# A tile of y kept in SBUF, and VectorE in GpSimd's place in the second layer: a float32 attention and two-layer kernel on one Trainium2 core

## What is computed

```python
scores = scale * np.matmul(q, k.transpose(0, 1, 3, 2))      # decayed causal attention, no softmax
attn = np.matmul(scores * Dmat, v)
x = attn.transpose(0, 2, 1, 3).reshape(2304, 512)
xn = x / rms(x) * rms_g                                     # first layer: 512 -> 1536 -> 512
g = xn @ w_gate
y = (g * sigmoid(g) * (xn @ w_val)) @ w_out
h = y @ w_in                                                # second layer: 512 -> 2048 -> 512
p = np.where(h >= 1, h, np.where(h <= -1, 0, (h + 1) ** 2 / 4))
out = p @ moe2_w_out
```

## Time and profile before

| | us |
|---|---|
| median of 3 runs | 904.11 |
| lowest and highest | 901.40, 905.42 |
| the profiled execution's own time | 900.61 |
| its span, from the first to the last instruction | 898.8 |
| TensorE matmul busy | 870.4 (97%) |
| VectorE, ScalarE, GpSimd busy | 571.9, 464.2, 251.9 |
| mean granted TensorE clock, share of full speed | 0.998 |

### The profile page before, as it was taken

One profiled execution on the slowest core, in us unless ns is written; L12 is line 12 of the kernel. 1 busy time (PEld: TensorE's weight loads), 2 busy tenths in 40 slices (PEclk: granted clock), 3 DMA queues, 4 the chain that ended last, 5 costly groups with the idle time before them and its releaser, 6 DMA issues.

```text
span 898.8 us, 17947 instructions
## 1 busy us (share of the span) xinstructions
PE 870.4 (97%) x7448; PEld 848.8 (94%) x7448; DVE 571.9 (64%) x799; ACT 464.2 (52%) x732; POOL 251.9 (28%) x172
## 2 busy tenths in 40 slices
PE   6898999999999999999999998999999999999998
PEld 5787999999999999999999988999999978999998
DVE  3599866477953653622242577766567879888884
ACT  2556654445654555511231457877778846433331
POOL 0236763446764664000040422404042000000000
PEclk9999999999999999999999999999999999999999
DMA  9984132333336336334633134233326673444442
GB/s 259 234 248 142 54 104 91 101 100 100 101 100 240 101 100 211 133 106 134 207 103 132 54 132 152 106 128 126 132 112 217 200 237 118 119 140 118 140 119 71
DMA packets 113329, 124.09 MB, mean 138 GB/s; under 512 B 6784, under 2 KB 85760, under 8 KB 113248
## 3 DMA queue, kind: packets, MB, share of 16 engines
q1 hardware_dynamic: 113248, 122.95, 43.5%
HBM read 80.45 MB, written 42.47 MB: 137 GB/s over the span
## 4 chain that ended last, share of the span: by engine, by line
PE 79%; DVE 7%; DMA 5%; ACT 3%; issue 2%; POOL 2%; SPq 1%; DVEq 0%; ACTq 0%
PE pair L727 14%; PE pair L729 14%; PE pair L728 14%; PE pair L825 6%; PE pair L827 6%; PE pair L826 6%; PE pair L888 5%; PE pair L890 5%; PE pair L889 5%; DMA a_kt<-ktok 4%; PE pair L858 1%; DVE cb L1496 1%; PE pair L859 1%; PE pair L860 1%; DVE wq L1528 1%
## 5 line engine op out<-in xcount | busy, mean ns | idle before, releaser
L727 PE MATMUL pair<-xc,wc 128*128 128x288 f32 x672 | 199.4, 297 | 0.6 <-ACT cp L1014 0.4
L728 PE MATMUL pair<-xc,wc 128*128 128x288 f32 x672 | 198.2, 295 | 0.0
L729 PE MATMUL pair<-xc,wc 128*128 128x288 f32 x672 | 197.6, 294 | 0.0
L1014 ACT ACTIVATE cp<-pair 128x576 f32<-128x576 f32 x160 | 103.4, 647 | 156.3 <-PE pair L729 150.2
L1679 POOL TENSOR_TENSOR wc<-wt,wc 128x512 fp32r<-128x512 f32 x84 | 122.6, 1483 | 92.2 <-ACT wc L947 86.6
L727 PE MATMUL pair<-xc,wr 128*128 128x288 f32 x448 | 133.6, 298 | 6.8 <-ACT cp L1014 6.3
L728 PE MATMUL pair<-xc,wr 128*128 128x288 f32 x448 | 132.2, 295 | 0.0
L729 PE MATMUL pair<-xc,wr 128*128 128x288 f32 x448 | 131.7, 294 | 0.0
L727 PEld LDWEIGHTS pair<-xc,wc 128*128 128x128 f32 x672 | 125.9, 187 | 1.6 <-issue 1.5
L729 PEld LDWEIGHTS pair<-xc,wc 128*128 128x128 f32 x672 | 126.6, 188 | 0.0
L728 PEld LDWEIGHTS pair<-xc,wc 128*128 128x128 f32 x672 | 126.2, 188 | 0.0
(11 more groups left out here) (124 smaller groups left out, 1702.6 us busy)
## 6 DMA issues: line engine op xcount, KB each, us to landing
b_scratch<-cb SPq DMA_DIRECT2D x32, 576.0 KB, 2.9
a_scratch<-cb SPq DMA_DIRECT2D x24, 576.0 KB, 2.9
av_r<-a_scratch SPq DMA_DIRECT2D x8, 1728.0 KB, 8.3
wt<-wB SPq DMA_DIRECT2D x72, 128.0 KB, 2.9
bt<-b_scratch SPq DMA_DIRECT2D x28, 256.0 KB, 2.8
bt<-b_scratch SPq DMA_DIRECT2D x56, 128.0 KB, 3.0
a_k<-kT SPq DMA_DIRECT2D x16, 288.0 KB, 8.0
a_q<-qT SPq DMA_DIRECT2D x16, 288.0 KB, 6.8
```

The lines of the kernel that those rows point to most:

```text
L727: pe.matmul(o, wh, xh, start=FIRST[i] and j == 0, stop=False, skip_group_check=True)
L728: pe.matmul(o, wh, xl, start=False, stop=False, skip_group_check=True)
L729: mm = pe.matmul(o, wl, xh, start=False, stop=j == 1, skip_group_check=True)
L1014: act.activation(copied(g, n)[:, :, :], pair[(X, Q, X, X)[n]][:, :, 0:HALF], ACT.Copy).then_inc(s_c, 1)
```

## The change

y goes from PSUM straight to its place `yr` in SBUF; the scratch tensor, the buffers `yo`, eight stores and four reloads are gone. For that the four tiles of y have their places in the second half of the first layer's weights, tile NT + 3 in the place of tile NT; the sums of tile NT + 2 go to where tile NT + 1 was; and tiles NT + 2 and NT + 3 exchange the places of their parts, with the order of the last four steps (`LAST_TILES`) following. Tile NT is combined before ht = 5 is copied out, in place of within it and after the next av, tile NT + 1 between ht = 6 and 7. The sums of tile NT + 2 are made ahead of ht = 7's copies, those of tile NT + 3 in step 0. From tile NT + 2 on and from unit 2UB + 1 on, all low parts that GpSimd made are VectorE's, the four plain blocks of the last product's first weights too. Cut to its core, in the order SP, ScalarE's copy (VectorE's changes likewise), ScalarE's y stage after `a_hi(6, 3)`, VectorE's after `a_lo(6, 3)`, the end of GpSimd's program:

```diff
+LAST_TILES = (0, 1, 3, 2)
...
-        xc_at = (z_xc, z_xc + XC, z_xc, z_xc + XC, z_xc, z_xc + XC, z_xc2, z_xc3)
+        xc_at = (z_xc, z_xc + XC, z_xc, z_xc + XC, z_xc, z_xc + XC, z_xc3, z_xc2)
-        xs = {T: place(f"xs{T}", [4, 2, HALF], z_x + (T - 2) * KB * SEQ * 4) for T in (2, 3)}
+        xs_at = {2: z_x, 3: z_x + KB * SEQ * 4, NT + 2: z_w + WU + KB * SEQ * 4}
+        xs = {T: place(f"xs{T}", [4, 2, HALF], o) for T, o in xs_at.items()}
-        yr_at = (z_w + WU, z_w + WU + KB * SEQ * 4, z_rest, z_w + WU)
-        yr = [place(f"yr{i}", [KB, SEQ], yr_at[i]) for i in range(NT)]
+        yr = [place(f"yr{i}", [KB, SEQ], z_w + WU + i % 3 * KB * SEQ * 4) for i in range(NT)]
...
-                if ht == 3:
-                    load_y(0)
-                if ht == 5:
-                    load_y(1)
-                store_y(ht)
...
-                    sp.wait_ge(s_y, KB * NHT)
-                    load_y(2)
-                    sp.wait_ge(s_xh, 7 * (NT + 1))
-                    sp.wait_ge(s_xlp, 3 * (NT + 1))
-                    sp.wait_ge(s_T, 4 * (NT + 1))
-                    load_y(3)
+                        sp.wait_ge(s_xld, 4 * (2 * NT - 1))
...
             def y_out(ht, m):
                 act.wait_ge(s_y, KB * ht + m + 1)
-                if ht > 1 and m == 0:
-                    act.wait_ge(d_ys[ht % 2], 16 * (ht // 2))
-                act.activation(yo[ht % 2][:, m, :], bank[(KB * ht + m) % 8][:, 0:HALF], ACT.Copy).then_inc(s_ye, 1)
+                if ht == 6 and m == 0:
+                    act.wait_ge(s_xh, 7 * (NT + 1))
+                    act.wait_ge(s_xlp, 3 * (NT + 1))
+                    act.wait_ge(s_T, 4 * (NT + 1))
+                act.activation(tokens(NT + ht // 2)[:, m, ht % 2 * HALF:(ht % 2 + 1) * HALF],
+                               bank[(KB * ht + m) % 8][:, 0:HALF], ACT.Copy).then_inc(s_ye, 1)
...
+            for i in range(4, 7):
+                unit_hi(2 * UB, i)
+            for i in range(4):
+                tile_hi(NT, i)
+            y_out(5, 0)
+            for i in range(4, 7):
+                tile_hi(NT, i)
+            y_out(5, 2)
+            for c in range(4):
+                a_hi(7, c)
+            y_out(6, 0)
+            y_out(6, 2)
+            for i in range(7):
+                tile_hi(NT + 1, i)
+            y_out(7, 0)
+            y_out(7, 2)
+            tile_hi(NT + 2, B11)
...
+            tile_sums(NT)
+            y_out(5, 1)
+            for i in T_BY_DVE:
+                tile_lo(NT, i)
+            y_out(5, 3)
+            for c in range(4):
+                a_lo(7, c)
+            y_out(6, 1)
+            y_out(6, 3)
+            tile_sums(NT + 1)
+            for i in T_BY_DVE:
+                tile_lo(NT + 1, i)
+            tile_sums(NT + 2)
+            y_out(7, 1)
+            y_out(7, 3)
+            for i in (B11, T1, B21):
+                token_lo(NT + 2, i)
...
             unit(2 * UB)
             tile(NT)
             tile(NT + 1)
-            tile(NT + 2)
-            tile(NT + 3)
-            for un in range(2 * UB + 1, UALL):
-                unit(un)
-            pool.wait_ge(s_wS, 4)
-            for n in range(4):
-                raw, hi, lo = w_plain(0, n)
-                pool.wait_ge(s_wAh, n + 1)
-                pool.tensor_tensor(lo, raw, hi.bitcast(F32), ALU.subtract).then_inc(s_wAp, 1)
```

More of the change, by code:

```diff
@@ L521, in load_b @@
                 T, r = QUARTERS[k]
-                last = GALL - NT + ((T + 1) * 2 * P - 1) // SEQ
+                last = ((T + 1) * 2 * P - 1) // SEQ
+                last = max(last_step(NT + n) for n in range(last + 1))
                 for g in (last - 1, last):
@@ L1161, in _ @@
                 copy(g, 0)
+                if n == 0:
+                    tile_hi(NT + 2, T1)
+                    tile_hi(NT + 2, B21)
                 if n:
                     parabola(g - 1, 0)
+                if n == 1:
+                    tile_hi(NT + 3, T2)
+                if n > 1:
                     parabola(g - 1, 1)
                 copy(g, 1)
+                if n == 0:
+                    for i in (T2, B22, T3):
+                        tile_hi(NT + 2, i)
                 if n == 1:
-                    tile_hi(NT + 3, B11)
+                    tile_hi(NT + 3, B22)
+                    tile_hi(NT + 3, T3)
+                    parabola(g - 1, 1)
                 if n == 3:
                     unit_hi(un + 1, A11)
-                if n:
+                if n > 1:
                     parabola(g - 1, 2)
@@ L1174, in _ @@
                 if n == 0:
-                    tile_hi(NT + 2, B11)
-                    tile_hi(NT + 2, T1)
+                    tile_hi(NT + 2, T4)
                 if n == 1:
-                    tile_hi(NT + 3, T1)
-                    tile_hi(NT + 3, B21)
+                    tile_hi(NT + 3, T4)
+                    parabola(g - 1, 2)
                 if n == 3:
@@ L1189, in _ @@
                 if n == 0:
-                    for i in (B21, T2, B22, T3, T4):
-                        tile_hi(NT + 2, i)
-                if n == 1:
-                    for i in (T2, B22, T3, T4):
+                    for i in (B11, T1, B21):
                         tile_hi(NT + 3, i)
@@ new lines, in _, with token_lo @@
+            tile_sums(NT)
[13 more added lines that the diff above has]
+            y_out(7, 3)
+            def token_lo(T, i):
+                if i in T_BY_DVE:
+                    tile_lo(T, i)
+                    return
+                dve.wait_ge(s_xh, 7 * T + i + 1)
+                dve.wait_ge(s_xlp, 3 * T + B_BY_POOL.index(i))
+                kk, th = {B11: (0, 0), B21: (1, 0), B22: (1, 1)}[i]
+                dve.tensor_tensor(xc[T][:, i, 1, :, :], part(tokens(T), kk, th),
+                                  xc[T][:, i, 0, :, :].bitcast(F32), ALU.subtract).then_inc(s_xlp, 1)
@@ L1493, in joined, with unit_lo @@
+            def unit_lo(un, i):
+                dve.wait_ge(s_wh, 7 * un + i + 1)
+                dve.wait_ge(s_wl, 7 * un + i)
+                if i == 0:
+                    dve.wait_ge(s_S, 4 * un + 4)
+                dve.tensor_tensor(w_part(un, i, 1), w_raw(un, i), w_part(un, i, 0).bitcast(F32),
+                                  ALU.subtract).then_inc(s_wl, 1)
             def joined(g, c):
@@ L1574, in _ @@
                 c11(g)
+                if n == 0:
+                    for i in (T2, B22, T3, T4):
+                        token_lo(NT + 2, i)
+                if n == 1:
+                    for i in (B11, T1, B21):
+                        token_lo(NT + 3, i)
                 if n:
                     joined(g - 1, 1)
+                if n == 1:
+                    token_lo(NT + 3, T2)
+                    token_lo(NT + 3, B22)
+                if n > 1:
                     joined(g - 1, 2)
-                if n in (0, 1):
-                    tile_sum(NT + 2 + n, T1)
-                    tile_sum(NT + 2 + n, T2)
                 if n in (GC - 3, GC - 1):
```

120 lines of the change are left out of this document (48 added, 72 removed).

## The result

| | before | after |
|---|---|---|
| median of 4 runs each | 903.3 us (901.4 to 905.42) | 893.39 us (891.68 to 896.08) |
| ratio, 95% interval | | 0.9877 [0.9848, 0.9906] |
| profiled execution, span | 900.61, 898.8 | 896.08, 894.3 |
| steps of the second layer, first to last | 189.10 | 181.05 |
| stage of y | 153.66 | 155.18 |

The change makes the kernel faster, as forecast, by a little over 1%; the interval of the ratio does not reach 1. It is more than the 8.5 us of the forecast: 9.9 us between the medians, 11.1 by the ratio. The profiled executions differ by only 4.5. The traces say which of these numbers belongs to the change.

A forecast was written before the change was run, and what follows sets the result against it. TensorE, busy 870.4 of 898.8 us, bounds the kernel; the second layer loses 9.90 us to stalls. Gains of 5.65 (steps 0 to 2) and 2.83 (unit changes) sum to 8.5, so 904.11 becomes 895.6; range 892.5 to 899.8.

The forecast's parts named there:

- Steps 0 to 2: Second layer's start: with the reload gone and sums made earlier, 6.57 us lost becomes 0.92, gain 5.65.
- Steps 7 and 11: Second layer's unit changes: c21 ends 2.41 us into step 7, the 1.04 lost goes, step 11 likewise; 2.08 together.
- The limit of 2.5: VectorE's work may end 2.5 us into the next step; from there each us late costs TensorE one.
- Step 4: Second layer's unit change: the 0.83 us lost goes, 0.08 added for the joint from step 3.
- Parts 1 and 2: Stage of y: y without memory (eight stores, four reloads gone) and tile NT made sooner; no cost.
- Part 5: Four lows of the last weights go to VectorE's step 14, 4 x 0.60 = 2.4 us; no cost.
- The sum: Whole kernel: 5.65 + 2.83 = 8.5 us gained; profiled execution 900.61 becomes 892.1.
- From the sum to the median: Whole time: the same 8.5 us taken off the three-run median 904.11 gives 895.6.
- The queue that runs over mildly: Rival, VectorE's queue: operations at 0.75 us instead of 0.67 lose 3.5 to 4 us of the gain, 899.3; 12%.
- The ring of waits: Rival, step 1: ScalarE's first copy and VectorE's sums still wait on each other; gain about 4 or 1 us; 8%.
- VectorE as the bound: Rival: 31 moved lows at 1.6 us each on VectorE cost 21 us against the 8.5, 917; decides from about 0.9; 3%.
- The rule of the Trainium skill: VectorE and GpSimd share a read port, so moving work might not help; part 4's 2.83 us would be about 0.

The follow-up runs named there:

- the six points: Changed kernel with c22 made twice in step 6 and three times in step 10, layer 183.31 us; read with other runs: c21's end against the step's loss.
- The two later comparisons: The changed kernel run again twice, no edit, against the kernel before: 897.93 us, ratio 0.9927, and 896.22 us, ratio 0.9922.

## Why the prediction was right, and where it was wrong

The mechanism held in the layer, 8.05 us gained for 8.48. The gain of the first comparison, 11.1 us by its ratio, lies beyond the forecast's bounds; the step that failed for it is the one from the sum to the median, and in the layer the step that failed is the spacing of the lows in step 4.

- **Steps 0 to 2: right in sum and in shape.** 6.57 to 0.92 was forecast, 0.91 is left (0.84 + 0.07). The hold in step 1 before copy 2 is there (product 5 starts at 541.80, 0.16 after it was due, forecast 0.17), c21 ends at 548.08, 2.40 us into step 2, where the layout gave 2.4, and c21 of step 0 ends 2.22 into step 1, where it gave 2.28. What was not seen is the slack in step 0, some 2 us of idle time on VectorE in the layout as in the trace.
- **What each edit brings was not forecast.** I had given all 5.65 to the reload that goes. The runs split it: y's way 3.13 and the tile lows 2.5. Without the move to VectorE, sums and combinations take 1.98 beside GpSimd and step 1 loses 3.36.
- **Steps 7 and 11: right.** c21 was to end 2.41 us into step 7 and ends at 2.42. The limit of 2.5 holds to within 0.1 at the six points, so "it just fits" was no luck.
- **Step 4: the mis-sized term.** Forecast 0.08, measured 0.53. The step that failed is "the five lows behind it are done 1.7, 1.5, 1.4 us and more before TensorE needs each". The 0.60 spacing that it rests on isn't theirs: it was read on two operations (L1523) that wait for high parts alone, and the lows that moved, each with a wait on the low before it, came 0.79 apart. Without the wait they come 0.60 apart and step 4 loses nothing. The loss stayed unseen because I asked whether TensorE gets the lows in time, and not who is queued behind them: the join, ScalarE's parabola behind it, and copy 2 behind that.
- **Parts 1 and 2, the stage of y: right, no cost.** 153.67 twice against 153.66. That tile NT is ready sooner brings nothing, as costed. The 155.18 of the first profile is the half-clock stretch. (The layout's 509.5 for the end of tile NT+1 is 0.7 more than its own terms, 499.7 + 5.4 + 3.75, give; measured it ends 9.5 us before step 0, forecast 9.3.)
- **Part 5: right.** The last product takes 187.50, 187.90 and 187.97 in the three profiles of the changed kernel, against 187.72.
- **The sum.** Layer gain 8.05 for 8.48. The forecast for the profiled execution (892.1, measured 896.08) missed by 4.0: 2.2 for a later start of the first layer, 1.5 for half clock, 0.4 for step 4.
- **From the sum to the median: the step that failed for the result.** "It lay 3.5 below the median of the three runs, 904.11; taking the same 8.5 off that gives 895.6": three runs don't fix a median when single runs of the kernel before go from 896.93 to 908.86, and "1.7 for the spread of three runs" was too little for two sides of four runs each. The first comparison's 893.39 is inside the range, but its ratio of 0.9877 says 892.2 of 903.3, below the low end of 892.5. The two later comparisons gave ratios that say 6.6 and 7.0 us, medians of 897.93 and 896.22, and 7.8 us with their runs pooled. So the miss is most likely the draw of eight runs, and that 893.39 came as near as it did to 895.6 is luck as well.
- **The rivals.** The queue that runs over mildly is the one that came true in step 4 alone (0.45 us, not 3.5), and for another cause than the 0.75 durations. The ring of waits is gone: ScalarE's copy 0 of step 1 (535.44) waits for TensorE alone. VectorE as the bound didn't come: a low costs it 0.60 to 0.79, below the 0.9 from which that decides. The rule of the Trainium skill named there (Perfetto Trace Analysis, Optimizing Scalar/DVE Operations), that moving work between VectorE and GpSimd might not help, did not hold here: moving it to VectorE is worth 2.4 and 2.5 us of the 8.05. VectorE is busy 65% of the time, and it is 11 us busier in all with the moved lows; on GpSimd they cost VectorE up to 1.2 us on an operation with two SBUF inputs that falls beside them, also at the one instant that TensorE waits for.

Open: the 3.13 is for the direct way, the places, the new order and the four lows of the last weights together. Of these the sooner tile NT and the sums ahead of the last copy each brought under 0.1 us in a run of its own. Whether storing and reloading y into a place of its own would have been enough for it was not tried. The kernel before has one profile, and its first layer starts earlier (89.11) than in any of the 13 profiles with the change (90.18 to 95.07), so no run shows whether the change delays that start. Nor is it known why the half-clock stretches fall where they do.

## What to carry to other kernels

Lay out both queues behind a moved operation by spacings, and follow each new entry to the instructions behind it on its own engine and across to the next one, not only to its reader; then find the one instant that may not be passed (here c21, 2.5 us into steps 2, 7 and 11, and sooner in step 1), since below it a delay costs nothing and above it every microsecond counts. GpSimd can be worth emptying even onto a busier VectorE, where VectorE's operations with two SBUF inputs stand in front of TensorE (1.85 to 1.99 us beside GpSimd, 0.75 alone). When an expected gain is about 1%, compare the stage's own length between profiles, and take the whole time from many runs.

## What was not expected of the hardware

- **A VectorE operation that waits on a semaphore of its own predecessor** starts about 0.79 us after it at 512 columns; without that wait 0.60. In a row of five, four such distances make 0.76 us.
- **Half-clock stretches that come in some executions and not in others.** In the first profile of the changed kernel TensorE drops to 1.2 GHz from 367.89 to about 371.3, 3.4 us, with matmuls back to back in it, 0.6 us after it had resumed from a wait of 1.91 us for av. All 14 profiles have that wait of 1.91 us; 6 of them have a half-clock stretch behind it, and a stage of y of 155.2 us, and the other 8, the kernel before among them, have full clock and 153.7. One stretch costs 1.5 us and is worth 0.002 of a run's mean clock (half of 3.4 us in 895); the steps of the table by mean clock are about as large or larger, 1.0 to 2.3 us where both rows have five runs or more.
- **The start of the first layer scatters**, 90.2 to 95.1 us over the 13 profiles with the change, whose attention code is the same.
